# Attention scores from split queries and keys, on one core: three rounded products in place of one exact one from the ninth pair group on

## The reference

```python
scores = scale * np.matmul(q, k.transpose(0, 1, 3, 2))
kth = np.partition(scores, -32, axis=-1)[..., -32:-31]
scores = np.where(scores >= kth, scores, -1e9)
attn = softmax(scores)
x = np.matmul(attn, v)                       # to (2304, 512)
h = x @ w_in;   x = np.maximum(0.01 * h, h) @ w_out        # 512 -> 2048 -> 512
h = x @ w_in2;  g = 0 below -1, h above 1, (h + 1)**2 / 4 between;  out = g @ w_out2
```

## Time and profile before

| | |
|---|---|
| median of 3 runs | 1202.3 us |
| profiled execution | 1198.35 us, span 1196.4 us, mean granted PE clock 0.973 |
| PE busy | 1108.2 us (93%), weight loads 999.2 us |
| DVE busy | 924.3 us (77%) |
| ACT busy | 701.0 us (59%) |
| POOL busy | 608.7 us (51%) |
| DMA | 287.12 MB, mean 240 GB/s |

### The profile page before, as it was taken

How to read it: one execution, slowest core, us unless ns; L and a number is a source line. 1 busy time by engine, 2 the same in 40 slices (tenths; PEclk the granted TensorE clock), 3 DMA queues, 4 the chain that set the end, 5 groups by cost and what they waited for, 6 DMA issues and landing times.

```text
span 1196.4 us, 21062 instructions
## 1 busy us (share of the span) xinstructions
PE 1108.2 (93%) x7360; PEld 999.2 (84%) x7360; DVE 924.3 (77%) x2088; ACT 701.0 (59%) x1579; POOL 608.7 (51%) x582
## 2 busy tenths in 40 slices
PE   3547998899999999999999989999899999999998
PEld 2335887778989988889987978998789999999998
DVE  7999999989799998998989999969989006300234
ACT  5676878756577765666666756566775424312232
POOL 5676778835366643655536744346644323222222
PEclk9758999989999999999999999999999999999999
DMA  6789997766667787767666756455356677787764
GB/s 228 280 300 342 348 346 285 270 229 206 220 223 233 255 285 257 275 230 258 236 233 211 249 182 222 159 198 175 121 194 217 201 256 250 252 283 251 250 239 150
DMA packets 86792, 287.12 MB, mean 240 GB/s; under 512 B 9632, under 2 KB 13472, under 8 KB 86688
## 3 DMA queue, kind: packets, MB, share of 16 engines
q1 hardware_dynamic: 79200, 270.04, 65.5%
q10 hardware_dynamic: 7488, 15.73, 3.9%
HBM read 247.46 MB, written 38.27 MB: 239 GB/s over the span
## 4 chain that ended last, share of the span: by engine, by line
PE 71%; DVE 19%; POOL 3%; issue 3%; ACT 3%; DMA 1%; POOLq 0%; SPq 0%; ACTq 0%
PE ps_f L812 19%; PE ps_f L820 19%; PE ps_f L813 18%; DVE top L1067 7%; DVE work L1070 7%; PE ps_av L771 6%; PE ps_s L727 3%; PE ps_t L748 2%; DVE drop L1076 2%; PE ps_t L727 2%; DVE part_r L1094 2%; PE ps_t L754 2%; POOL gate L644 1%; POOL drop L630 1%; POOL part_o L650 1%
## 5 line engine op out<-in xcount | busy, mean ns | idle before, releaser
L1067 DVE MAX8 top<-work 128x8 f32<-128x576 f32 x432 | 309.3, 742 | 0.1
L812 PE MATMUL ps_f<-xy,w_ring 128*128 128x384 f32 (+2 forms) x896 | 288.8, 322 | 4.5 <-ACT xy L994 2.5
L820 PE MATMUL ps_f<-gate,w_ring 128*128 128x384 f32 (+2 forms) x896 | 281.3, 314 | 9.5 <-POOL gate L644 9.4
L812 PE MATMUL ps_f<-gate,w_ring 128*128 128x384 f32 (+2 forms) x896 | 286.0, 319 | 1.0 <-ACT part_o L975 0.6
L630 POOL TENSOR_TENSOR drop<-scores,drop 128x576 f32<-128x576 f32 x144 | 207.9, 1444 | 150.1 <-DVE drop L1076 150.1
L820 PE MATMUL ps_f<-xy,w_ring 128*128 128x384 f32 (+2 forms) x896 | 280.8, 313 | 1.8 <-POOL xy L654 1.6
L813 PE MATMUL ps_f<-xy,w_ring 128*128 128x384 f32 (+2 forms) x896 | 280.1, 313 | 0.0
L813 PE MATMUL ps_f<-gate,w_ring 128*128 128x384 f32 (+2 forms) x896 | 280.0, 312 | 0.0
L1070 DVE MATCH_REPLACE8 work<-top,work 128x576 f32<-128x576 f32 x288 | 212.7, 739 | 0.0
L812 PEld LDWEIGHTS ps_f<-xy,w_ring 128*128 128x128 f32 x896 | 169.7, 189 | 20.5 <-issue 9.3
L644 POOL TENSOR_TENSOR gate<-part_r,gate 128x384 fp32r<-128x384 f32 (+2 forms) x112 | 101.5, 909 | 157.4 <-ACT gate L979 157.2
(11 more groups left out here) (83 smaller groups left out, 1822.0 us busy)
## 6 DMA issues: line engine op xcount, KB each, us to landing
w_ring<-w_split SPq DMA_DIRECT2D x412, 512.0 KB, 4.2
w_split<-w_ring SPq DMA_DIRECT2D x36, 512.0 KB, 6.0
raw<-wd SPq DMA_DIRECT2D x64, 256.0 KB, 4.3
w_split<-xy SPq DMA_DIRECT2D x28, 512.0 KB, 3.7
kq<-kqd ACTq DMA_DIRECT2D x12, 576.0 KB, 5.8
v_sb<-vd ACTq DMA_DIRECT2D x12, 320.0 KB, 3.2
out_t<-y_acc ACTq DMA_DIRECT2D x12, 192.0 KB, 3.6
kq<-kqd SPq DMA_DIRECT2D x3, 576.0 KB, 6.7
```

Source lines behind the costliest of these rows:

```text
L812: pe.matmul(out, w[:, 0, m], high, start=first, stop=False)
L820: mm = pe.matmul(out, w[:, 0, m], low, start=False, stop=end)
L1067: dve.max(top[:, t % T_SLOTS, 8 * r:8 * r + 8], source(t, r)).then_inc(dve_step, 1)
```

## The change

Three things, in the program's own words:

- From `gp` 8 on (`FIRST_ROUNDED`), `score` makes three products of split queries and keys, high by high, low by high and high by low, from `kq_split`, in place of one fp32 product of `kq`. Mixed items, in all groups, now load 128 columns of weights for both heads and write all partitions of the tile; the layout in DRAM is padded for that.
- `kq` has two slots (`KQ_SLOTS`), filled by SP per group and pair: 832 columns for a group of two items, 960 for one of three. ACT loads no more queries and keys.
- ACT rounds the high part (`high_kq`) at the end of step n-2, and GpSimd subtracts the low part (`low_kq`) in two halves in step n-1: the first at the head of the step, the second behind its mask. PE's first score of the group waits for both.

```diff
+Q_COLS = 2 * P + REST
+KQ_COLS = Q_COLS + S + REST
+KQ_SLOTS = 2
+FIRST_ROUNDED = 8
...
+KQ_FREE = [score_step(ITEMS[FIRST_OF_GROUP[gp]]) if gp >= FIRST_ROUNDED else
+           score_step(ITEMS[LAST_SCORED[gp]]) + 1 for gp in range(GROUPS)]
+KQ_LOAD_AT = {KQ_FREE[gp - KQ_SLOTS]: gp for gp in range(KQ_SLOTS, GROUPS)}
+KQ_NEEDED = {score_step(ITEMS[FIRST_OF_GROUP[gp]]): gp for gp in range(FIRST_ROUNDED, GROUPS)}
...
-        kq = sb("kq", [P, PAIRS, 2 * S])
+        kq = sb("kq", [P, KQ_SLOTS, KQ_COLS])
+        kq_split = sb("kq_split", [P, 2, KQ_COLS], F32R)
...
-            def load_kq(b, pair):
-                sp.dma_start(kq[:, pair, :], kqd[b * PAIRS + pair, :, :]).then_inc(kq_loaded[pair], 16)
+            def load_kq(gp):
+                old = gp - KQ_SLOTS
+                if old >= FIRST_ROUNDED:
+                    sp.wait_ge(kq_low_done, 2 * (old - FIRST_ROUNDED + 1))
+                elif old >= 0:
+                    sp.wait_ge(scores_done, 2 * LAST_SCORED[old] + 2)
+                first, end = kq_span(gp)
+                sp.dma_start(kq[:, gp % KQ_SLOTS, first:end], kqd[gp, :, first:end]).then_inc(kq_loaded[gp % KQ_SLOTS], 16)
...
             for s in range(len(PLAN)):
+                if s in KQ_LOAD_AT:
+                    load_kq(KQ_LOAD_AT[s])
...
+            def low_kq(gp, part):
+                pool.wait_ge(kq_high_done, gp - FIRST_ROUNDED + 1)
+                first, end = kq_parts(gp)[part]
+                pool.tensor_tensor(kq_split[:, 1, first:end], kq[:, gp % KQ_SLOTS, first:end],
+                                   kq_split[:, 0, first:end].bitcast(F32), ALU.subtract).then_inc(kq_low_done, 1)
...
+                if s + 1 in KQ_NEEDED:
+                    low_kq(KQ_NEEDED[s + 1], 0)
                 for u in first:
                     event(u)
                 if READY[0] <= s < TILES + MASK_LAG:
                     mask(s - MASK_LAG)
+                if s + 1 in KQ_NEEDED:
+                    low_kq(KQ_NEEDED[s + 1], 1)
                 for u in second:
                     event(u)
...
+                elif it.gp >= FIRST_ROUNDED:
+                    pe.wait_ge(kq_low_done, 2 * (it.gp - FIRST_ROUNDED + 1))
...
+                    high, low = kq_split[:, 0, :], kq_split[:, 1, :]
+                    terms = [(high, high), (low, high), (high, low)]
...
+                    for n, (q, k) in enumerate(terms):
+                        start, stop = n == 0, n == len(terms) - 1
+                        pe.matmul(out[:, 0, 0:PART], q[0:D, rows[0]], k[0:D, even:even + PART], start=start, stop=stop)
+                        mm = pe.matmul(out[:, 1, 0:PART], q[D:P, rows[1]], k[D:P, odd:odd + PART], start=start, stop=stop)
+                    mm.then_inc(scores_done, 1)
...
-                if it.mixed and it.b + 1 < B:
-                    act.dma_start(kq[:, it.pair, :], kqd[(it.b + 1) * PAIRS + it.pair, :, :]).then_inc(kq_loaded[it.pair], 16)
+
+            def high_kq(gp):
+                act.wait_ge(kq_loaded[gp % KQ_SLOTS], 16 * ((gp + 1) // KQ_SLOTS))
+                if gp > FIRST_ROUNDED:
+                    act.wait_ge(scores_done, 2 * LAST_SCORED[gp - 1] + 2)
+                first, end = kq_span(gp)
+                act.activation(kq_split[:, 0, first:end], kq[:, gp % KQ_SLOTS, first:end], ACT.Copy).then_inc(kq_high_done, 1)
...
+                if s + 2 in KQ_NEEDED:
+                    high_kq(KQ_NEEDED[s + 2])
```

More of the change, by code:

```diff
@@ L235, in score_step, with kq_span, kq_parts @@
     return max(it.first - it.mixed, READY[0] + it.n - FIRST_LATE)
+FIRST_OF_GROUP = [min(it.n for it in ITEMS if it.gp == gp) for gp in range(GROUPS)]
+LAST_SCORED = [max(it.n for it in ITEMS if it.gp == gp) for gp in range(GROUPS)]
 SCORED_AT = {s: [it for it in ITEMS if score_step(it) == s] for s in range(ATTENTION_STEPS + 1)}
 OUT_AT = {out_step(it): it for it in ITEMS}
+KQ_FREE = [score_step(ITEMS[FIRST_OF_GROUP[gp]]) if gp >= FIRST_ROUNDED else
+           score_step(ITEMS[LAST_SCORED[gp]]) + 1 for gp in range(GROUPS)]
+KQ_LOAD_AT = {KQ_FREE[gp - KQ_SLOTS]: gp for gp in range(KQ_SLOTS, GROUPS)}
+KQ_NEEDED = {score_step(ITEMS[FIRST_OF_GROUP[gp]]): gp for gp in range(FIRST_ROUNDED, GROUPS)}
 VALUES_AT = {values_step(gp): gp for gp in range(GROUPS)}
+def kq_span(gp):
+    return (Q_COLS - GROUP_WIDTH[0], Q_COLS + S) if gp // PAIRS % 2 == 0 else (0, KQ_COLS)
+def kq_parts(gp):
+    first, end = kq_span(gp)
+    middle = (first + end) // 2
+    return (first, middle), (middle, end)
 def waits_for(u, before):
@@ L461, in build @@
         kq_first = sem("kq_first")
-        kq_loaded = [sem("kq_loaded%d" % p) for p in range(PAIRS)]
+        kq_loaded = [sem("kq_loaded%d" % a) for a in range(KQ_SLOTS)]
+        kq_high_done = sem("kq_high_done")
+        kq_low_done = sem("kq_low_done")
         v_loaded = [sem("v_loaded%d" % p) for p in range(PAIRS)]
@@ L571, in stream @@
                              w_dram[STREAM[g], :, :, :]).then_inc(w_loaded[g % W_SLOTS], 16)
-            sp.dma_start(kq[:, 0, S:2 * S], kqd[0, :, S:2 * S]).then_inc(kq_first, 16)
-            sp.dma_start(kq[:, 0, 0:2 * P], kqd[0, :, 0:2 * P]).then_inc(kq_first, 16)
+            first, end = kq_span(0)
+            sp.dma_start(kq[:, 0, Q_COLS:end], kqd[0, :, Q_COLS:end]).then_inc(kq_first, 16)
+            sp.dma_start(kq[:, 0, first:Q_COLS], kqd[0, :, first:Q_COLS]).then_inc(kq_first, 16)
             load_raw(0)
-            load_kq(0, 1)
-            sp.dma_start(kq[:, 0, 2 * P:S], kqd[0, :, 2 * P:S]).then_inc(kq_loaded[0], 16)
+            load_kq(1)
             for j in range(1, RAW_SLOTS):
@@ L716, in score @@
                     pe.wait_ge(kq_first, 32)
-                elif it.rows == 2 or it.rows == 0 and it.gp:
-                    pe.wait_ge(kq_loaded[it.pair], 16 * (it.b + 1))
+                elif it.gp >= FIRST_ROUNDED:
+                    pe.wait_ge(kq_low_done, 2 * (it.gp - FIRST_ROUNDED + 1))
+                elif it.gp and it.n == FIRST_OF_GROUP[it.gp]:
+                    pe.wait_ge(kq_loaded[it.gp % KQ_SLOTS], 16 * ((it.gp + 1) // KQ_SLOTS))
                 need(pe, scores_copied, 2 * it.n)
@@ L721, in score @@
                     need(pe, p_t_copied, ITEMS_OUT[it.n])
-                q, k = kq[:, it.pair, 0:S], kq[:, it.pair, S:2 * S]
-                for j, out in enumerate(score_halves(it)):
[L724 to L738, removed]
@@ new lines, in score @@
+                if it.gp < FIRST_ROUNDED:
+                    exact = kq[:, it.gp % KQ_SLOTS, :]
+                    terms = [(exact, exact)]
+                else:
+                    high, low = kq_split[:, 0, :], kq_split[:, 1, :]
+                    terms = [(high, high), (low, high), (high, low)]
+                first = it.col + Q_COLS - GROUP_WIDTH[it.group]
+                rows = slice(first, first + P), slice(first, first + P)
+                if it.mixed:
+                    rows = rows[0], slice(first + REST - P, first + REST)
@@ new lines, in score @@
+                for j, out in enumerate(score_halves(it)):
+                    even, odd = Q_COLS + j * PART, Q_COLS + j * PART + (REST if it.mixed else 0)
+                    for n, (q, k) in enumerate(terms):
[3 more added lines that the diff above has]
+                    mm.then_inc(scores_done, 1)
@@ L1213 @@
     kt = k.transpose(0, 1, 3, 2).reshape(B * PAIRS, 2, D, S)
-    odd = np.concatenate([kt[:, 1, :, MAIN:], kt[:, 1, :, :MAIN]], axis=2)
-    kt = np.stack([kt[:, 0], odd], axis=1)
-    kqd = np.concatenate([qt, kt], axis=3).reshape(B * PAIRS, P, 2 * S)
+    odd = np.concatenate([kt[:, 1, :, MAIN:], kt[:, 1, :, :MAIN], kt[:, 1, :, MAIN:]], axis=2)
+    kt = np.stack([np.concatenate([kt[:, 0], np.zeros_like(kt[:, 0, :, :REST])], axis=2), odd], axis=1)
+    kt, qt = kt.reshape(B, PAIRS, P, S + REST), qt.reshape(B, PAIRS, P, S)
+    groups = [np.concatenate([np.zeros_like(qt[..., :REST]), qt[..., :2 * P], kt], axis=3),
+              np.concatenate([qt[..., 2 * P:], kt], axis=3)]
+    kqd = np.stack(groups, axis=1).reshape(GROUPS, P, KQ_COLS)
     vh = v.reshape(B * PAIRS, 2, S, D)
```

2 lines of the change are left out of this document (removed).

## The result

The change makes the kernel slower: 1240.93 us, median of 4 runs (1240.32 to 1241.96), beside 1202.74 us of the kernel before on the same chip, a ratio of 1.0316 [1.0299, 1.0334] and 38.2 us more. 1209.8 us were predicted, with a range up to 1223. The profiled execution took 1240.88 us, its span is 1239.1 us.

A forecast was written before the change was run, and what follows sets the result against it. The prediction took the chain of waits as the bound, mostly PE, with DVE from 640 to 720 us. Stops 13.9 plus DVE 1 less saving 7.4 gave +7.5 us on the median 1202.3: 1209.8 us, range 1199 to 1223.

The forecast's parts named there:

- GpSimd's work beside the wait: 48 subtractions on GpSimd, 55 us in all against 343 us free; charged only through the score's wait and DVE.
- The other four (40, 67, 84, 103): Stops at first scores in these steps, counted at nothing: an earlier stop held PE back, or PE waits soon after.
- the ten: The ten of 24 groups where PE was expected to reach the first score too early, about 33 us in sum.
- The stops kept, 13.9 us: PE's waits for GpSimd's halves at first scores, as far as they were expected to stay: 13.9 us together.
- The six steps: First scores at steps 36, 57, 62, 72, 108 and 134, whose stops were counted, together 13.9 us.
- The half clock: Long stops may lower PE's clock, about 1.6 us per slow stretch; outside the sum, with 4.8 us in the range.
- DVE, 1 us: DVE's mark of dropped columns and like operations, perhaps slower beside GpSimd: 1 us on the path, between 0 and 3.
- The saving, 7.4 us: Six single passes replace four in PE's score items: 0.16 us per item, 46 items on the path, 7.4 us won.
- ACT's copies, loads, SP's queue at nothing: ACT's rounding copies (27 us), more DMA loads and their move to SP's queue, all counted at no time on the path.
- the first two: Rivals: stops only replace later waits, 1195.9 us, chance 0.17; about half is taken up, 1202.9 us, chance 0.15.
- the first one: Rival: PE's stops at scores only take the place of later waits, 1195.9 us; chance 0.17.
- The third: Rival: PE's score passes do not get shorter, loads or head halves coming one after the other, 1237.4 us; chance 0.06.

The follow-up runs named there:

- the unused split: Changed kernel with the split still made by ACT and GpSimd, but PE takes raw queries and keys as exact products and does not wait; 1218.35 us, ratio 1.0126.
- the short halves: Changed kernel with GpSimd's two operations cut to 16 columns each, PE still waiting, low parts left out of the scores; 1212.96 us, ratio 1.0090.
- ACT's copy only: Changed kernel without GpSimd's halves: PE waits for ACT's rounded copy, which all three products take; 1197.60 us, ratio 0.9960.

## Why the prediction was wrong

The sign and the place were right: PE idle ahead of the first scores, ended by GpSimd's split, the longest at 36, 62 and 108; the second half right behind the mask; the products 0.13 us apart; the tail of unchanged length. The stops came to 46.3 us, above the 20 to 35 expected. The size was off by 31 us, and two terms failed: GpSimd's work beside the wait was put at nothing and cost 15.3 us, and of the stops 13.9 us were kept where the runs show about 28. By its own steps:

- **"The other four (40, 67, 84, 103) I count at nothing: an earlier stop has held PE back already."** This step failed. PE stops there for 12.8 us (2.9, 2.9, 3.3, 3.7), and they lose 14.4, of which 1.9 are spread; 98 and 139, which were not among the ten, lose 6.4. A stop gave PE no lead for the next one: DVE's marks fall behind with PE. Around step 62 PE's units fall 6.2 us further behind the execution before, the marks around step 67 5.2, so the mask ahead of the next first score is late by as much. But the stops are not what most of this loss needs: with no score waiting the unused split loses 12.0 us at these four (3.3 of them, at 40 and 103, show without any split too), and the short halves, which still stop PE there for 7.2 us, lose 1.9.
- **The stops kept, 13.9 us.** The six steps lose 22.9: 3.3 (2.1 predicted), 0.3 (1.9), 6.9 (4.0), 3.5 (2.1), 8.2 (2.5), 0.7 (1.3). At 62 I took the mask's end from the trace before and added one half of 1.23 us; the stop is 5.6 us, for the mark that the mask waits for had fallen 10.3 us behind the trace before, PE's units only 8.8, and the half took 1.46. The first half, ahead of that mask, was done before the mark came. At 108, 2.0 us of PE's later wait were to take up a part; nothing was taken up, that wait is still 1.98 us. At 134 it was: PE stops for 5.1 us, its later wait of 2.62 us is gone, and 0.7 us are lost.
- **GpSimd's work beside the wait.** This step failed too. I set its 55 us against 343 us free and charged it only to the score (and 1 us to DVE). The unused split shows 15.3 us that have nothing to do with the score's wait: where a join stood behind the split, ACT already waited for it, and the copy behind it in ACT's order came just in time for PE's transposes. Split by the runs, the 38.2 us are 15.3 for the work, 9.9 for the waits in their places less the saving, and 13.0 that appear only with both, when PE waits through the halves' own length (46.3 us instead of 27.3). The last is a remainder; no run shows it by itself. The waits alone, against the run with ACT's copy only, are 15.4, so with the remainder the stops come to about 28.
- **The half clock, left out of the sum.** The range held two or three more slow stretches, 4.8 us; there were ten more. The products of the units lie 14.5 us further apart, 4.2 in the run with ACT's copy alone; about 10 of the 38 us go this way. No run took the stops away and kept the clock low, so this is worked out from rows.
- **DVE, 1 us.** DVE's busy time rose by 18 us, so this term was far too small as a count. Yet in the groups without joins the unused split lost nothing, so little of it can have been on the path; this is argued, not tested. That the mark stands behind GpSimd, which I had left open, is so (last section).
- **The saving, 7.4 us.** 4.5 us at the eleven groups of the rest, 27 items, 0.17 us each (0.16 predicted); 5.4 us in the whole time with ACT's copy alone. Right in size.
- **ACT's copies, loads, SP's queue at nothing.** The first held as work, the others within 2.3 us.

Of the rivals, the first two fell with the stops that added up; what the first one says happened at 134 alone. The third gave 1237.4 us, near the result, but that is chance, for its mechanism fell: the passes did get shorter.

## What to carry to other kernels

Here work added to GpSimd, which is idle 44% of the stretch, cost time only near operations that another engine was already waiting for. Before work is put on an engine with idle time, look for the waits that the engine ends today, even those of one microsecond on an engine off the path, and follow the waiting engine's queue to what PE needs next. When stops are priced from the trace before, let the whole pipeline slip: a stop also delayed the producers that feed the next one, so the sum of the stops (33 us here) was a better guess than letting the first pay for the later ones (13.9). And before an addition is judged by what waits for it, run it once with nobody waiting.

## What was not expected of the hardware

DVE's mark of the dropped columns takes 0.51 us where no GpSimd operation lies beside it. In the changed kernel 20 marks begin inside a GpSimd operation (at least 0.05 us behind its start and 0.2 ahead of its end), and every one of them ends 0.31 to 0.32 us behind that operation's end; in the kernel before all 13 such marks do. One that began with a split, from the timelines of DVE and GpSimd:

```profile
560.13 1.52 DVE L1130 TENSOR_SCALAR drop<-scores,top 128x576 f32<-128x576 f32 x1
...
560.12 1.21 POOL L693 TENSOR_TENSOR kq_split<-kq,kq_split 128x480 fp32r<-128x480 f32 x1 [4.00 <-ACT kq_split L959]
```

The mark began 0.01 us behind the split and ended 0.32 us behind its end. MAX8 and MATCH_REPLACE8 keep their time: the runs' means are 742 to 746 and 738 to 743 ns. The Trainium skill, SBUF — State Buffer, section SBUF: two separate sides, says that DVE operations in a mode with two ports, or with two inputs from SBUF, and GpSimd's lock each other out of a shared pair of ports for a whole instruction; the rows agree for the mark, though what is left of it behind the other's end is less than its own 0.51 us, and the search shows no such lock.
